# First loads and constants reordered, products of ones on TensorE, and the second expert's routing moved earlier, in an attention + routed experts + feed-forward kernel

## The reference

```python
# 1. attention with a sigmoid: 4 batches, 12 heads, 448 positions, 64 per head
scores = q @ k.T / sqrt(64) - log(448)
x = (1 / (1 + exp(-scores))) @ v              # -> (1792, 768)

# 2. eight experts with a capacity of 224 tokens, filled by the best scores first
logits = x @ w_gate                           # (1792, 8)
for idx in argsort(-logits.flatten()):        # token tok, expert e
    if tok has an expert or e has 224 tokens: continue
    assigned[tok] = e
for e in range(8):
    out[assigned == e] = relu(x[assigned == e] @ w1[e]) @ w2[e]   # 768 -> 1024 -> 768

# 3. feed-forward with a PReLU of its own slope for each column
h = out @ w_in                                # 768 -> 2048
y = (max(h, 0) + alpha * min(h, 0)) @ w_out   # 2048 -> 768
```

## Time and profile before

| | |
|---|---|
| Runs | 1060.93, 1059.88, 1057.77 us; median 1059.88 |
| Profiled execution | 1057.56 us, span of the core's instructions 1055.9 us |
| TensorE | busy 971.5 us (92% of the span), mean granted clock 0.970 |
| VectorE, ScalarE, GpSimd busy | 568.7 (54%), 393.4 (37%), 187.3 (18%) |
| Chain that ended last | TensorE 84%, VectorE 9%, ScalarE 3%, DMA 1% |

### The profile page before, as it was taken

The page is one execution under the profiler, slowest core; times in us unless marked ns, Lnnn a source line. Parts: engine busy times, 40 slices in busy tenths (PEclk is TensorE's granted clock), DMA queues, the critical chain, the costliest instruction groups (busy, mean ns, idle before and its releaser), DMA issues.

```text
span 1055.9 us, 16340 instructions
## 1 busy us (share of the span) xinstructions
PE 971.5 (92%) x6340; PEld 837.9 (79%) x6340; DVE 568.7 (54%) x1289; ACT 393.4 (37%) x629; POOL 187.3 (18%) x202
## 2 busy tenths in 40 slices
PE   4999999806979999899999999999999999999994
PEld 3555555406969898799989998998999999999993
DVE  3344443597566827956953685596448546211110
ACT  3767766501042223355322214542121355222212
POOL 0010011105160010244301014350101326000001
PEclk9999999956989999999999999999999999999998
DMA  9899998407289685956877855579695446966501
GB/s 199 222 265 269 270 265 250 156 17 254 72 236 371 205 225 179 296 133 211 291 283 234 245 169 131 199 233 347 233 243 190 151 123 197 380 231 214 179 1 52
DMA packets 121474, 222.30 MB, mean 211 GB/s; under 512 B 51424, under 2 KB 69216, under 8 KB 121408
## 3 DMA queue, kind: packets, MB, share of 16 engines
q1 hardware_dynamic: 88064, 120.34, 36.7%
q0 software_dynamic: 21280, 91.59, 28.1%
q10 hardware_dynamic: 12064, 9.47, 3.6%
HBM read 184.84 MB, written 36.52 MB: 210 GB/s over the span
## 4 chain that ended last, share of the span: by engine, by line
PE 84%; DVE 9%; ACT 3%; issue 1%; DMA 1%; POOL 1%; ACTq 0%; POOLq 0%; DVEq 0%
PE psum L907 19%; PE psum L895 19%; PE psum L842 11%; PE psum L872 11%; PE psum L644 8%; PE psum L628 7%; DVE hits L1406 4%; PE psum L837 2%; PE psum L612 2%; PE psum L867 2%; PE psum L655 1%; DMA stage<-x_rows,tok_idx 1%; DVE unit L1306 1%; PE psum L789 1%; PE psum L663 1%
## 5 line engine op out<-in xcount | busy, mean ns | idle before, releaser
L907 PE MATMUL psum<-g_high,unit 128*128 128x448 f32 x768 | 231.1, 369 | 4.3 <-DVE g_low L1334 4.1
L895 PE MATMUL psum<-y_high,unit 128*128 128x448 f32 x768 | 230.8, 368 | 4.4 <-ACT below L1041 4.3
L907 PEld LDWEIGHTS psum<-g_high,unit 128*128 128x128 f32 x768 | 144.3, 188 | 18.9 <-DVE g_low L1334 7.7
L895 PEld LDWEIGHTS psum<-y_high,unit 128*128 128x128 f32 x768 | 144.3, 188 | 17.8 <-ACT below L1041 5.8
L907 PE MATMUL psum<-g_low,unit 128*128 128x448 f32 x384 | 140.3, 365 | 0.0
L895 PE MATMUL psum<-y_low,unit 128*128 128x448 f32 x384 | 140.2, 365 | 0.0
L1306 DVE TENSOR_TENSOR unit<-raw,unit 128x768 fp32r<-128x768 f32 (+1 forms) x106 | 109.3, 1060 | 40.3 <-ACT unit L1014 34.9
L1040 ACT ACTIVATE above<-psum 128x448 f32<-128x448 f32 x64 | 34.9, 545 | 248.6 <-PE psum L895 248.6
L1329 DVE SCALAR_TENSOR_TENSOR below<-below,neg_alpha,above 128x448 f32<-128x448 f32 x64 | 43.8, 684 | 146.7 <-ACT below L1041 146.6
L842 PE MATMUL psum<-x_high,unit 128*128 128x224 f32 x672 | 119.4, 279 | 3.0 <-DVE unit L1306 3.0
L872 PE MATMUL psum<-h_high,unit 128*128 128x224 f32 x672 | 115.7, 276 | 1.4 <-issue 1.4
(11 more groups left out here) (168 smaller groups left out, 1260.2 us busy)
## 6 DMA issues: line engine op xcount, KB each, us to landing
unit<-ffn_parts SPq DMA_DIRECT2D x120, 768.0 KB, 5.7
ffn_parts<-pre_parts POOLq DMA_DIRECT2D x24, 768.0 KB, 6.2
ffn_parts<-unit SPq DMA_DIRECT2D x8, 768.0 KB, 5.4
q_in<-in_q_dram SPq DMA_DIRECT2D x24, 224.0 KB, 4.4
k_in<-in_k_dram SPq DMA_DIRECT2D x24, 224.0 KB, 6.1
v_in<-in_v_dram SPq DMA_DIRECT2D x24, 224.0 KB, 6.8
x_rows<-x_tok POOLq DMA_DIRECT2D x8, 672.0 KB, 5.5
rank_in<-suit_flat POOLq DMA_DIRECT2D x6, 896.0 KB
```

What stands on the lines that cost most here:

```text
L895: last = pe.matmul(psum[:, IN_BANK, 0:PAIR], w, y[:, c, :], start=(c == 0 and i == 0), stop=(c == DC - 1 and i == 2))
L907: last = pe.matmul(psum[:, OUT_BANK + d, 0:PAIR], w, g[:, m % 2, :], start=(m == 0 and i == 0), stop=(m == FC - 1 and i == 2))
```

## The change

It touches three places.

The start: SyncE's loads of the first batch are unrolled, without waits for the first three pairs; v of a pair is issued behind q and k of the next; the first k is issued by ScalarE. VectorE writes `ones_f` and `gate_bias` first, makes `ident` next, splits the first two pairs of q and k, and only then computes the other constants. TensorE runs 12 products of ones (float32, 128x128), then waits for `ident` instead of `const_done`, and makes the first scores of pair 0 before it transposes pair 1. ScalarE runs a one-column sigmoid first, and the first sigmoids ahead of rounding pair 1.

Round 0 of the routing: `keep_busy(n)` puts n products of ones (bf16, 112x448, into a bank that is free) ahead of `spread_thr(0)` (122), `sum_flags(0)` (9), `sum_idx(0)` (11) and `turn_suit(1)` (9). GpSimd gathers the token rows behind two units of w1 instead of four.

Round 1: the three products stand ahead of steps 7, 8 and 10, `turn_first(1)` ahead of step 13, and ScalarE and VectorE round and split expert 1's first two units at step 12 and the next two at step 13, where all were done at step 14 before. GpSimd gathers the token rows behind three units of w1 instead of four, and loads suitabilities at other places.

```diff
+    FILLERS = 12
+    BUSY_SEARCH, BUSY_FLAGS, BUSY_PLACES, BUSY_VALUES = 122, 9, 11, 9
...
+        FIRST_AT = OWN - 1
+        def prepared(s):
+            return {OWN - 2: OWN + 2, OWN - 1: OWN + 4}.get(s, 0) if s < OWN else s + LEAD + 1
...
-                THR_AT[r], FLAGS_AT[r], IDX_AT[r] = 9, 10, 13
+                THR_AT[r], FLAGS_AT[r], IDX_AT[r] = 7, 8, 10
...
+            def load_qk(b, hp, first):
+                n = pair(b, hp)
+                if not first or n >= RING:
                     sp.wait_ge(qk_turned, turned(n - RING, 1))
+                sp.dma_start(q_in[hp % RING][:], pair_rows(q, b, hp)).then_inc(qk_loaded[hp % RING], 16)
+                if not first or n > 0:
+                    sp.dma_start(k_in[hp % RING][:], pair_rows(k, b, hp)).then_inc(qk_loaded[hp % RING], 16)
...
+                for hp in range(PAIRS + 1):
+                    if hp < PAIRS:
+                        load_qk(b, hp, first)
+                    if hp > 0:
+                        load_v(b, hp - 1, first)
...
+            gather_w1(0, range(2))
+            gather_x(0)
+            gather_w1(0, range(2, DC))
+            gather_w2(0)
+            gather_w1(1, range(3))
+            gather_x(1)
+            gather_w1(1, range(3, DC))
+            store_suit(2)
+            gather_w2(1, range(3))
+            spread_suit(2)
+            gather_w2(1, range(3, EC))
...
-            pe.wait_ge(const_done, 1)
+            pe.wait_ge(ones_done, 1)
+            for i in range(FILLERS):
+                pe.matmul(psum[:, i % JT, 0:128], ones_f[:], ones_f[:], start=True, stop=True)
+            pe.wait_ge(ident_done, 2)
             turn_qk(0, 0)
+            score(0, 0, 0)
             turn_qk(0, 1, second=True)
-            score(0, 0, 0)
             score(0, 0, 1)
...
+            def keep_busy(n):
+                for _ in range(n):
+                    pe.matmul(psum[0:P, Y_BANK, 0:4 * P], ones_b[:], ones_b[:].unsqueeze(1).to_broadcast([P, 4, P]),
+                              start=True, stop=True)
...
-                if s == OWN:
+                if s == FIRST_AT:
                     turn_first(1)
...
+            keep_busy(BUSY_SEARCH)
             spread_thr(0)
+            keep_busy(BUSY_FLAGS)
             sum_flags(0)
+            keep_busy(BUSY_PLACES)
             sum_idx(0)
+            keep_busy(BUSY_VALUES)
             turn_suit(1, range(G))
...
+            act.dma_start(k_in[0][:], first_k).then_inc(qk_loaded[0], 16)
...
-            act.wait_ge(const_done, 1)
+            act.wait_ge(ones_done, 2)
+            act.activation(counts[:], ones_f[:, 0:1], ACT.Sigmoid)
...
-                round_units(0 if s < OWN else s + LEAD + 1)
+                round_units(prepared(s))
...
+            dve.memset(ones_f[:], 1.0).then_inc(ones_done, 1)
+            dve.memset(gate_bias[:], -float(np.log(S))).then_inc(ones_done, 1)
...
+            dve.wait_ge(diff_done, 1)
+            dve.tensor_copy(iota_f[:, I_DIFF:I_DIFF + 128], iota_i[:, I_DIFF:I_DIFF + 128]).then_inc(ident_done, 1)
+            dve.wait_ge(ident_done, 1)
+            dve.tensor_scalar(ident[:], iota_f[:, I_DIFF:I_DIFF + 128], 0.0, None, ALU.is_equal).then_inc(ident_done, 1)
...
-                    split_units(0 if s0 < OWN else s0 + LEAD + 1)
+                    split_units(prepared(s0))
```

More of the change, by code:

```diff
@@ L1285, in _ @@
                     split_qk(0, hp, i, second=(hp == 1))
+            dve.wait_ge(iota_done, len(IOTAS) - 1)
+            for at, n, _, _, _ in IOTAS:
+                if at != I_DIFF:
+                    last = dve.tensor_copy(iota_f[:, at:at + n], iota_i[:, at:at + n])
+            last.then_inc(const_step, 1)
+            dve.tensor_scalar(expert_i[:], iota_i[:, I_COL:I_COL + 33], 4, 1, ALU.logical_shift_right,
+                              ALU.bitwise_and).then_inc(const_step, 1)
+            dve.wait_ge(const_step, 2)
@@ new lines, in _ @@
+            dve.wait_ge(digit_step, len(SHIFTS) - WEIGHED)
+            for i in range(len(SHIFTS) - WEIGHED):
+                dve.tensor_scalar(by_digit[:, i, 0:32:DIGIT], same_expert[:, 0:32:DIGIT], MAGIC, None, ALU.mult).then_inc(digit_step, 1)
+            dve.wait_ge(digit_step, 2 * (len(SHIFTS) - WEIGHED))
+            for i in range(2):
+                dve.memset(same_expert[:, DIGIT * i:DIGIT * i + 1], 0.0)
+            dve.tensor_copy(place_f[:], place_i[:]).then_inc(const_step, 1)
+            dve.wait_ge(const_step, 6)
@@ L1286, in _ @@
+            dve.tensor_copy(count_down[:], iota_f[:, I_DOWN:I_DOWN + E])
+            dve.tensor_copy(slot_row[:], iota_f[0:P, I_SLOT:I_SLOT + P])
+            dve.tensor_copy(w1_row0[:], iota_f[:, I_W:I_W + DC])
+            dve.tensor_copy(w2_row0[:], iota_f[:, I_W:I_W + EC])
+            for i in range(3):
+                last = dve.tensor_copy(token_parts[:, :, i], iota_f[0:P, I_TOK + i * G:I_TOK + (i + 1) * G])
             work_on(0, 0, True, False)
```

138 lines of the change are left out of this document (53 added, 85 removed).

## The result

| | before | after |
|---|---|---|
| Median of 4 runs | 1060.41 us | 1049.36 us (1048.26 to 1050.24) |
| Ratio of the times, 95% interval | | 0.991 (0.989 to 0.992) |
| Profiled execution's span | 1055.9 us | 1048.6 us |
| TensorE busy, mean granted clock | 971.5 us, 0.970 | 996.9 us, 0.989 |
| Expert 1's first product starts | 301.30 us | 284.12 us |

The change makes the kernel 10 to 11 us faster (11.05 by the medians, 10.0 by the ratio; 7.3 between the two profiled spans, which are single executions). 1038 was forecast, with a range of 1032 to 1045: right in sign, and half the forecast gain is missing. In the profile, the gain is 17.2 us when expert 1 starts and only 7.6 us when the feed-forward starts 44 us later.

A forecast was written before the change was run, and what follows sets the result against it. TensorE was taken as the bound: its work plus holes at the start and between some 209 and 301 us. Start 6.9 plus middle 14.5 gave 21.4 us off the 1059.88 median, so 1038 us; range 1032 to 1045.

The forecast's parts named there:

- Start: Kernel start: 2.6 us from table loads, 2.3 from an earlier first transpose, 2.0 from the clock; 6.9 us gained.
- the clock term: Kernel start: products of ones raise TensorE's clock, so scores and transposes run faster; 2.0 us taken, bounds 0 and 2.9.
- Ones of the routing: Round 0's search: 122 products hidden or at most 0.4 us late, other groups costed at nothing; round 1's search 1.6 us earlier.
- the rival of half-clock ones: Round 0's search: products of ones run at half clock and thresholds wait behind them; 1068 us, chance 0.04.
- Expert 0: Middle: token rows land sooner, start near 248.3 us, first product 18.3 us, step 7 at 268.9, TensorE then waiting 1.6 us.
- rival (a): Between round 0's last ones and expert 0's products the clock falls back; 1.7 us lost, 1040 us, chance 0.15.
- The middle's gain: Routing up to expert 1's first product: start 12.0 us earlier, product 2.5 us shorter; 14.5 us, bounds 12 to 16.5.
- Behind it each routing duty is tied to a step and moves along: After expert 1's first product: later routing work shifts earlier with TensorE's steps, so the 14.5 us stay; no cost given.
- (b): Kernel start stays bound by loads and half clock, first transpose at 7.3; 2.8 us less gain, 1041 us, chance 0.08.
- (c): Token-row gathers keep their 7.4 us despite fewer units ahead; expert 1 starts 2.6 us later, 1042 us, chance 0.05.
- (d): Round 0's search: the products of ones run at half clock, the 122 taking 49.5 us; slower, 1068 us, chance 0.04.
- (e): Whole change does not take hold, an overlooked wait keeping the starts; same time within 0.3% (3.2 us), chance 0.02.

## Why the prediction was wrong

**Start, forecast 6.9 us: right.** 7.6 us in the trace, 8.4 by the medians of the kernel with the start alone. Table loads and first transpose (6.45 for 6.5) as forecast; the clock term was put at 2.0, and the kernel without the twelve products gives 2.6 in its trace. Pair 2's split and pair 0's v were covered.

**Ones of the routing: right in the changed kernel's profile.** The 122 are hidden, 0.190 us each, and the rival of half-clock ones fell. That they would move little was in the sum too: the search of round 1 was costed 1.6 us earlier (1.9 came), and the experiment without them shows nothing that a timing can tell. But the last nine are not always hidden, as the forecast had it: in two of the variants' traces (the load behind all eight, and no first products) they ran at half speed and stood in the chain for 3.4 and 3.2 us.

**Expert 0: partly wrong.** It starts at 242.27, 1.6 us later than the forecast's 248.3 less the start's 7.6. The second gather was issued 2.45 us behind the tokens' numbers (1.6 forecast) and landed in 4.56 (4.63); 1.56 us lay between its landing and expert 0, where 0.6 was forecast. Then rival (a) came in: the clock fell for 243 to 246 us and the first product took 20.08 instead of 18.3. TensorE reached step 7 1.8 us behind VectorE instead of 1.6 before it. The last row gather took 4.47 us, 0.80 of which TensorE waited. Together expert 1 starts at 284.12 and not at 281.7; its product is 16.07 long, as forecast. The middle's gain up to its end is 12.1 us in place of 14.5, within its bounds of 12 to 16.5. Rival (a) so makes most of these 2.4 us in the trace, and was priced at 1.7; yet the kernel whose trace has no fall of the clock is not measurably faster, as VectorE stands right behind. As the fall comes at different places in different traces, that (a) came in here is partly chance.

**"Behind it each routing duty is tied to a step and moves along": this step failed.** It took everything behind expert 1's first product as a shift at no cost, and 12.1 us of the 19.7 were lost there. Three things were wrong in it.

The load for round 2 was not tied to TensorE's steps but stood in GpSimd's queue, and the change itself moved it, from behind six units to behind three; I named the move in the text of the change and gave it no price. A load does not get faster when TensorE does: with TensorE 17 to 20 us ahead, the 15 us which the fourth unit of w2 took were no longer covered. And a unit that TensorE does not need yet can still stop it, since ScalarE rounds six units of w2 ahead of the first product's result. The profile of before held the price of the load: at 306.51, with the next unit rounded at 320.73.

That the load's place makes the hole is shown: put back it removes the hole, the same place costs nothing in the kernel before, and another queue does not cure it. That the wait runs through ScalarE's order is read from the program and from four traces; no run changed that order.

With the place alone mended, a second wait, round 2's early passes on VectorE before expert 1's split, took most of the rest (1045.3), and with both mended the time is 1041.7: 17.5 us below its own kernel before, against 21.4 forecast. Its trace is 20.6 us ahead at the feed-forward's start, so nearly all of the forecast is reached there, and the missing 3 us lie behind it, in a part of the kernel for which the forecast had no term.

**Rivals.** (b) start bound by loads with half clock: no (6.45, not 7.3). (c) 7.4 us gathers: no, 4.5. (d), (e): no. None of the five had a wait behind expert 1. The sign was right for the start's sake: the kernel with only the start reaches 1050.5, the whole change 1049.4.

**The range.** Its bounds do not follow from its own terms: 4.1 + 12 and 8.3 + 16.5 us below 1059.88 are 1043.8 and 1035.1, not 1043 and 1034, and the bounds of the middle, 12 and 16.5, are stated without their working. Neither is what made it miss.

**The signs.** One table load, first transpose, scores and the threshold product of round 0 (226.11, directly behind VectorE) came as listed. VectorE idled 2.16 us for round 1's thresholds, not under 1, and TensorE did not idle at step 7. Expert 1's first product came 21.5 us after those thresholds instead of 19, and was 16.07 us long. One of the things that were to prove the forecast wrong did happen, in small: TensorE waited 0.80 us for token rows at step 13. The large one was not on the list: "it would be wrong if" looked at ones, rows and attention, and not at weights.

## What to carry to other kernels

When a change pulls one engine ahead by some 20 us, price each transfer whose result that engine takes in the next 20 us: its issue may move along with the engine, its length does not, and the trace of before has that length. A transfer that the diff moves past others in a queue gets a price even when it looks like a detail of placement. Then read what each engine's program puts ahead of the result that the next one needs: a transfer needed only later can stand there. And when the first wait is mended, look at what stands next before judging the mending: here the place of the load alone gave some 4 us by the ratios, and with the passes behind it 7.

## What the hardware showed that I had not expected

- A load in which 16 partitions each read the same 7 KB row passed 161 to 209 GB/s while the 16 DMA engines were full (share 0.94 to 1.10), in the changed kernel, the kernel before and both kernels with an extra load; with it on SyncE's queue and more gathers beside it they passed 229 and 243, and once it had landed 342 to 402. 896 KB of it, with gathers beside them, kept the next gather waiting for 13 to 15 us, from another queue some 12 us at the median.
- With plain rows of 7 KB in its place, full engines passed 230 to 307 GB/s (288 to 294 us in the kernel with separate rows): less than afterwards, more than with the spread rows. One trace.
- In the first 20 us the profile's granted clock reads 1.00, while products run at half speed: the window below, of the kernel before, holds the scores that take 2.63 us instead of 1.40. There the length of a product tells the speed, not that column (the one before DMA share and GB/s).

```profile
18.00:22.00 4.00, 3.11 (x15) 2.26 (x16) 0.00 (x0) 1.33 (x2) 0.00 (x0) 1.00 1.20 255
```
